# Retention and two expert layers on one core: the first state sums before the query table, and four loads and sums at other places

## The reference

```python
scores = scale * np.matmul(q, k.transpose(0, 1, 3, 2))       # 8 batches, 8 heads, 576 tokens, 64 features
Dmat = np.where(rel >= 0, gamma[:, None, None] ** rel[None, :, :], 0.0)
x = np.matmul(scores * Dmat[None, :, :, :], v)               # -> (4608, 512)
h = np.maximum(np.maximum(x @ w1, x @ w2), x @ w3)           # 512 -> 768
x2 = h @ w_out                                               # 768 -> 512
a, b = x2 @ u1, x2 @ u2                                      # 512 -> 1024
out = (a * b @ u3) @ u_out                                   # 1024 -> 1024 -> 512
```

## Time and profile before

| | |
|---|---|
| time, median of 3 runs | 1230.83 us (1230.39 to 1232.71) |
| profiled execution, its own time | 1231.38 us |
| its span, first to last instruction | 1229.5 us |
| busy | PE 99%, DVE 60%, ACT 40%, POOL 35% of the span |
| matmuls | 8594 |
| bytes moved | 169.55 MB, 138 GB/s over the span |

### The profile page before, as it was taken

One profiled execution on the slowest core, in us unless ns is written; L12 is line 12 of the kernel. 1 busy time (PEld: TensorE's weight loads), 2 busy tenths in 40 slices (PEclk: granted clock), 3 DMA queues, 4 the chain that ended last, 5 costly groups with the idle time before them and its releaser, 6 DMA issues. The chain is left out here.

```text
span 1229.5 us, 21665 instructions
## 1 busy us (share of the span) xinstructions
PE 1222.1 (99%) x8594; PEld 1202.2 (98%) x8594; DVE 737.7 (60%) x1065; ACT 485.7 (40%) x781; POOL 433.3 (35%) x234
## 2 busy tenths in 40 slices
PE   9999999999999999999999999999999999999999
PEld 8899999999999999999999999999999999999998
DVE  6444648845545464668886777454545466786653
ACT  3433544523232232326655544242323234554441
POOL 3535528220201102053867761202020217366550
PEclk9999999999999999999999999999999999999999
DMA  9999934121203021054464441313131342444441
GB/s 346 337 337 353 336 125 146 52 78 38 92 26 104 26 70 60 34 173 144 152 228 171 160 157 52 104 52 110 52 116 53 109 179 96 154 155 161 159 157 65
DMA packets 87332, 169.55 MB, mean 138 GB/s; under 512 B 9272, under 2 KB 58680, under 8 KB 87232
## 3 DMA queue, kind: packets, MB, share of 16 engines
q1 hardware_dynamic: 87232, 168.17, 39.1%
HBM read 106.27 MB, written 61.87 MB: 137 GB/s over the span
## 5 line engine op out<-in xcount | busy, mean ns | idle before, releaser
L1261 PE MATMUL ps<-chi,whi 128*128 128x384 f32 x2016 | 674.4, 335 | 1.9 <-ACT w L931 0.7
L1263 PE MATMUL ps<-chi,wlo 128*128 128x384 f32 x2016 | 673.5, 334 | 0.0
L1262 PE MATMUL ps<-clo,whi 128*128 128x384 f32 x2016 | 673.4, 334 | 0.0
L674 POOL TENSOR_TENSOR raw<-raw,raw 128x768 f32<-128x768 f32 (+3 forms) x102 | 268.1, 2650 | 582.8 <-DMA raw<-xd 203.5
L1261 PEld LDWEIGHTS ps<-chi,whi 128*128 128x128 f32 x2016 | 378.4, 188 | 4.5 <-ACT w L931 1.4
L1262 PEld LDWEIGHTS ps<-clo,whi 128*128 128x128 f32 x2016 | 378.4, 188 | 0.0
L1263 PEld LDWEIGHTS ps<-chi,wlo 128*128 128x128 f32 x2016 | 378.4, 188 | 0.0
L940 DVE TENSOR_TENSOR clo<-raw,chi 128x768 fp32r<-128x768 f32 (+2 forms) x168 | 253.5, 1537 | 41.7 <-ACT chi L851 41.7
L851 ACT CAST chi<-raw 128x768 fp32r<-128x768 f32 (+2 forms) x168 | 180.1, 1081 | 90.5 <-PE ps L1263 48.1
L931 ACT COPY w<-ps 128x384 f32<-128x384 f32 x126 | 60.5, 480 | 238.4 <-PE ps L1263 237.0
L918 ACT COPY u<-ps 128x384 f32<-128x384 f32 x126 | 60.7, 482 | 160.5 <-PE ps L1263 158.9
(11 more groups left out here) (61 smaller groups left out, 820.7 us busy)
## 6 DMA issues: line engine op xcount, KB each, us to landing
gd<-h SPq DMA_DIRECT2D x96, 192.0 KB, 1.9
raw<-gd SPq DMA_DIRECT2D x24, 768.0 KB, 6.3
qks<-qk SPq DMA_DIRECT2D x30, 576.0 KB, 7.3
hd<-h SPq DMA_DIRECT2D x72, 192.0 KB, 1.9
raw<-hd SPq DMA_DIRECT2D x24, 576.0 KB, 6.6
x2d<-h SPq DMA_DIRECT2D x48, 192.0 KB, 2.9
raw<-x2d SPq DMA_DIRECT2D x24, 384.0 KB, 4.5
outT<-h SPq DMA_DIRECT2D x48, 192.0 KB, 1.9
```

The lines of the kernel that those rows point to most:

```text
L674: return nc.gpsimd.tensor_tensor(out_, a, b, op)
L1261: nc.tensor.matmul(to, w1, x1, start=(start and k == 0), stop=False, skip_group_check=True)
L1262: nc.tensor.matmul(to, w1, x2, start=False, stop=False, skip_group_check=True)
L1263: last = nc.tensor.matmul(to, w2, x1, start=False, stop=(k == KH[st] - 1), skip_group_check=True)
```

## The change

Five edits, of which the first is in the first part and the others in the matrix stages:

1. At the start PE sums the states of pair 0 right behind the scores of pair 0 and `decay_powers`; `query_powers` comes behind them, behind a wait for the masked decay table, and writes to another PSUM bank. Of the zero products 8 stand before (9 earlier), 2 (7 earlier) before the scores of pair 1, and none (2 earlier) between these and `sum_state(1)`. The scores of pair 1 don't wait for `qtab` any more.
2. The first tile of stage C is loaded in unit 48 instead of 47, behind the stores of the results of unit 47.
3. The sums of weight 11 are made in unit 57 instead of 56, and its casts and subtractions likewise.
4. The first tile of stage I is loaded in the middle of unit 64 and not at its end. It waits block by block for the low halves of the last tile of C, not for all of them; POOL gets one wait for that.
5. Block 0 of the second tile of stage O is loaded at the end of unit 113 and not in unit 114.

```diff
-...10: 52, 11: 56, 12: 59, 13: 63, ...
+...10: 52, 11: 57, 12: 59, 13: 63, ...
...
-for _wi, _it, _later in ((9, 52, 0), (11, 56, 2), (12, 60, 2), (13, 64, 2)):
+for _wi, _it, _later in ((9, 52, 0), (11, 57, 2), (12, 60, 2), (13, 64, 2)):
...
+I_OVER = {0: 0, 3: 2, 6: 4, 2: 1}
...
-        _a = {C: 47, I: None, O: 107}[_st]
+        _a = {C: 48, I: None, O: 107}[_st]
...
-                if t == 0:
+                if t == 0 and st == I:
+                    sp.wait_ge(combined, 4 * tau)
+                elif t == 0:
                     sp.wait_ge(c_lo, 7 * tau)
...
+                    if t == 0 and st == I:
+                        sp.wait_ge(c_lo, 7 * (tau - 1) + I_OVER[pos] + 1)
...
+                        if it == 64:
+                            load_raw(I * TILES)
...
-                            load_raw(tau, (0, 3, 6, 2) if tau // TILES == C else (0, 3, 2))
+                            load_raw(tau, (0, 3, 6, 2) if tau // TILES == C else (3, 2))
...
+                if it == FIRST_UNIT[O] - 1:
+                    load_raw(O * TILES + 1, (0,))
...
-                if it == 64:
-                    load_raw(I * TILES)
...
+                    if tau == I * TILES:
+                        pool.wait_ge(c_lo, 7 * (tau - 1) + 4)
...
-                if n == 1:
-                    pe.wait_ge(qtab_made, 1)
...
-            run_idle(9, S_WC)
+            run_idle(8, S_WC)
...
-                        query_powers()
-                        run_idle(4, 3)
-                        sum_state(0)
-                        run_idle(3, 3)
+                        sum_state(0)
+                        pe.wait_ge(dec_made, 1)
+                        query_powers()
+                        run_idle(2, 3)
                     if n == 1:
-                        pe.wait_ge(dec_made, 1)
-                        run_idle(2, S_WC)
                         pe.wait_ge(state_made, NC)
                         sum_state(1)
+                        pe.wait_ge(qtab_made, 1)
                         run_idle(2, S_WC)
```

More of the change, by code:

```diff
@@ L141 @@
              18: 69, 19: 109, 20: 111}
-W_SUM_AT = {2: 0, 3: 1, 4: 2, 5: 3, 6: 4, 7: 5, 8: 6, 9: 50, 10: 52, 11: 56, 12: 59, 13: 63, 14: 66, 15: 67, 16: 68,
+W_SUM_AT = {2: 0, 3: 1, 4: 2, 5: 3, 6: 4, 7: 5, 8: 6, 9: 50, 10: 52, 11: 57, 12: 59, 13: 63, 14: 66, 15: 67, 16: 68,
             17: 69, 18: 70, 19: 110, 20: 112}
@@ L856, in _ @@
             act.wait_ge(qtab_powers, 1)
-            nc.scalar.copy(qtab[:, :], ps[:, 2, :]).then_inc(qtab_made, 1)
+            nc.scalar.copy(qtab[:, :], ps[:, S_WC, :]).then_inc(qtab_made, 1)
             decay_values(1)
@@ L1210, in query_powers @@
             def query_powers():
-                nc.tensor.matmul(ps[:, 2, :], pows[:, 2 * P:3 * P], pows[:, 3 * P:], start=True, stop=True,
+                nc.tensor.matmul(ps[:, S_WC, :], pows[:, 2 * P:3 * P], pows[:, 3 * P:], start=True, stop=True,
                                  skip_group_check=True).then_inc(qtab_powers, 1)
             pe.wait_ge(idle_zeroed, 1)
-            run_idle(9, S_WC)
+            run_idle(8, S_WC)
             pe.wait_ge(zeroed, 10)
```

## The result

| | before | after |
|---|---|---|
| time, median | 1231.62 us (1230.39 to 1232.71, 4 runs) | 1245.33 us (1243.61 to 1245.79, 4 runs) |
| ratio, 95% interval | | 1.0110 (1.0095 to 1.0125) |
| profiled execution: its time, its span | 1231.38, 1229.5 us | 1243.61, 1241.8 us |

The changed kernel is 13.7 us slower. The forecast was 1237.8 us with a range up to 1241.0: the sign was right, the size too small by 7.5 us.

A forecast was written before the change was run, and what follows sets the result against it. PE, busy 99% of the 1229.5 us span, bounds the kernel, so only its gaps count. Terms -0.8 - 0.35 + 1.5 + 6.4 + 1.9 - 0.9 - 0.6 = +7.15 gave 1238.0, stated as 1237.8 us, range 1233.0 to 1241.0.

The forecast's parts named there:

- Edit 3: Stage C, copy w of unit 57: weight 11's sums behind tile 8's combinations make PE wait; +6.4 us, bounds +4.4 to +12.
- The clock: Behind edit 3's gap: PE, after standing still 7.3 us, may restart at the slow clock; +1.9 us, bounds 0 to 4.1.
- The rival that the clock stays: Behind edit 3's gap: the clock stays up, all else as forecast; 1236.0 us, chance 0.17.
- The row that the term was taken from: Program start: first 18 zero products took 0.23 us each, later ones 0.13, read as 1.2 and 2.4 GHz.
- Edit 2: Stage C: gap at 531.60 goes, -0.35 us; late weight 9 makes a new gap ending with copy u, +1.5 us.
- Edit 4: Start of stage I: tile 12's loads come some 7 us sooner, so the gap at 699.09 goes; -0.9 us.
- Edit 1: Program start: fewer zero products bring the scores of pair 1 sooner; -0.8 us, gain bounded by 0 and 1.75.
- Edit 5: Stage O, tile 19: one block less ahead of POOL's start shortens the gap at 1084.18; -0.6 us, at worst nothing.
- My own sum of edit 2: Weight 10's sums on POOL, stage C: beside DVE, four sums can lose up to 3.2 us through the shared port.
- its bound of 0: Stage O, edit 5: at worst the earlier load of block 0 of tile 19 gives nothing.
- The gain of 0.6: Stage O: the gap of 0.53 us at 1084.18 goes with its slow matmul, -0.6 us.

The follow-up runs named there:

- b_e3: The kernel before with edit 3 alone; 1238.11 us, ratio 1.0059.
- a_fill: The changed kernel with 36 matmuls of 128x384 added ahead of PE's wait for the copy w of unit 57; 1242.53 us, ratio 1.0086, in two groups.
- b_e5: The kernel before with edit 5 alone; 1231.74 us, ratio 1.0005.
- a_145: The changed kernel with edits 2 and 3 undone, so edits 1, 4 and 5 without an extra wait on POOL; 1234.49 us, ratio 1.0022.
- a_t6back: The changed kernel with edit 2 undone (tile 6 loaded in unit 47 ahead of the stores); 1242.75 us, ratio 1.0079.
- a_blk0back: The changed kernel with edit 5 undone (block 0 of tile 19 loaded in unit 114); 1241.64 us, ratio 1.0075.
- a_w11back: The changed kernel with edit 3 undone (sums, casts and subtractions of weight 11 at unit 56 again); 1236.42 us, ratio 1.0039.
- a_castonly: The changed kernel with the sums of weight 11 back in unit 56, its casts and subtractions still in unit 57; 1242.08 us, ratio 1.0084.
- a_w9first: The changed kernel with weight 9 loaded directly ahead of tile 6 in unit 48, not behind it; 1242.65 us, ratio 1.0087.

## Why the prediction was right in sign and wrong in size

- **Edit 3, right.** Chain, place and releaser are as forecast: issue of tile 8 to POOL's start 5.6 us forecast, 5.35 in b_e3 and 6.0 in after; four combinations 12.8 forecast, 12.75 measured. The sums were mis-sized: 1.05 us each was read from weight 10, whose tiles are 128x384; those of weight 11 are 128x256 and took 0.72. That is 1.3 us of the 6.4, and the ledger has 5.5.
- **The clock, right, and too small.** +1.9 forecast, 2.5 measured; a_fill shows that the slow matmuls are the clock's and not late operands. The rival that the clock stays is out for the gap of edit 3: seven traces have it at 4.6 us or more, with slow matmuls behind it each time. The row that the term was taken from is not one of the clock, though: the record of the granted clock begins at 4.91 us in before, behind the slow products of the earlier trace rows, so that their cause isn't shown. The Trainium skill, "TensorE: Matmul & The Clock Gate", in the part on the clock gate, has half rate as the state of an idle engine. The windows behind the gap of edit 3 agree.
- **Edit 2, mechanism right, size too small.** The gap stands where it was forecast, ended by copy `u`. Weight 9 landed 2.9 us later, not 4.3; POOL's sums of weight 10 lost 2.5 us beside DVE. The loss per sum had been read too small, for 1.85 and 1.05 us are of two sizes: the size of the 1.85 takes 0.72 undisturbed. And besides the gap of 1.14 us there are others, which made it 2.7 instead of 1.5.
- **Edit 4, the number right by luck.** The loads do come 7.4 us sooner against PE than in the three later traces without the edit (7 were forecast), and the gaps are gone in every trace with the edit. But three of four traces without it have no gap at 699 either, so the 0.9 us were mostly a mark of one execution; 0.3 us at 703 are what edit 4 can be seen to win. The profile names no engine for the end of that gap, and it was put down to the first blocks of stage I without being shown.
- **Edit 1, open.** The median of the thirteen traces has the scores of pair 1 at 10.04, 0.6 us sooner than before. The sum gave 0.8 us to the end; the median of 11 runs shows 0.5, with an interval that holds no change.
- **Edit 5, the step that failed.** The prediction said "one block less in front of it is worth about 2 us there" and "both can give nothing at worst". It did start POOL sooner, by 4.4 us against PE. What I didn't ask is what POOL's instruction would then run beside. My own sum of edit 2 used the mutual hold of POOL and DVE, but only as something that POOL loses. Here DVE lost, and PE waits for DVE: its subtraction went from 2.28 to 5.57 us. 4.5 of the 5.4 us that separate the ledger's sums are this term, and its bound of 0 was wrong. The gain of 0.6 was no better: the gap at 1084 is missing in the four other traces without the edit. The rows were there: DVE's subtraction at 1062.77 and POOL at 1066.27, 3.5 us apart, before an edit that draws POOL forward by more than that.
- **Open.** Why SP took 1.78 us for one store in b_e5, and why that store's issue differs between kernels, isn't shown. In the two traces it decided whether edit 5 cost 5 us or nothing; why the executions of b_e5 nearly all were cheap and those of a_145 mostly dear is not known. That the two groups of a_fill are this race is argued from one trace, not shown for the unprofiled executions.

## What to carry to other kernels

An instruction's start is an event that others can lose to: before a load is moved forward, look at what the engine behind it would then run beside, and whether PE waits for that neighbour. Where two engines hold each other, order them with a wait or cut the long instruction into pieces; either gave back 5 to 6 us here, more than any of the moves was meant to win. And an edit undone that gives back the forecast number proves little without its trace, as a_t6back showed.

## What the runs showed of the hardware

- The wait for the shared pair is not shown as idle time but as a longer instruction: 5.57 us instead of 2.28 for the same subtraction, with no releaser named. A group's mean duration hides it; instructions of one form have to be compared one by one.
- In one case (a_t6back) a lead of 0.05 us was enough. The loser waits to the other's end.
- An engine can lose the pair between two of its own instructions that follow without a pause: POOL's record in after begins inside DVE's subtraction before, is 0.82 us longer than the same instruction's 3.50 in a_blk0back, and ends ahead of DVE's next.
- The clock fell behind gaps in PE of 6.5, 3.5 and once 2.4 us, and it cost 2.5, 1.6 and 1.6 us. It doesn't always: behind the gap of 3.5 us in a_w11back the matmuls start 0.17 us apart from 1071.18 on, while behind a gap of that length they turned slow in after, a_145, a_castonly, a_t6back and a_w9first. Behind another gap of 2.3 us it did not fall either. Where it fell, it could be after PE had started again: in a_145 PE starts at 1067.02, and the first distance of 0.32 us is at 1068.50. The windows of a_t6back behind its gap at 578 and of a_castonly behind its gap at 640:

```profile
581.00:585.30 4.30, 4.30 (x16) 4.30 (x17) 3.58 (x3) 1.53 (x2) 4.30 (x2) 0.60 0.67 221
```

```profile
642.00:646.00 4.00, 3.81 (x20) 3.44 (x21) 4.00 (x4) 1.94 (x3) 3.92 (x3) 1.00 0.85 280
```
